# Attention, Fourier mixing and two MLPs on one core: some low-part subtractions change engine, and the first stage gets a new order

## The reference

```python
# 1. attention in chunks of 32 queries: 16 keys to the left, 32, 8 to the right, 8 memory keys; 8 heads of 64
scores = scale * np.matmul(q_c, k_full.transpose(0, 1, 3, 2))
scores = scores - np.max(scores, axis=-1, keepdims=True)
a = np.exp(scores)
a = a / (np.sum(a, axis=-1, keepdims=True) + 1e-09)
out[:, :, c_start:c_end] = np.matmul(a, v_full)
# 2. Fourier mixing and a channel MLP (d_model 512, hidden 2048)
mixed = np.real(fft(fft(x, axis=1), axis=2)).astype(np.float32)
u = x + mixed
un = (u - mu) / np.sqrt(var + 1e-06)
x = u + np.maximum(un @ w_ch1, 0.0) @ w_ch2
# 3. gated MLP with a convolution of 3 taps over the tokens (hidden 1024)
h = np.maximum(x @ w_in, 0.0)
return (h * sigmoid(conv3(h, conv_w))) @ w_out
```

## Time and profile before

| | |
|---|---|
| median of 3 runs | 959.13 us (956.21 to 959.7) |
| the profiled execution | 955.41 us, its span 953.6 us |
| PE busy | 923.5 us, 97% of the span |
| DVE, ACT, POOL busy | 679.6 us (71%), 419.3 us (44%), 178.3 us (19%) |
| chain that ended last | PE 86%, DVE 5%, DMA 3%, ScalarE 1%, GpSimd 1% |

### The profile page before, as it was taken

How to read it: one execution, slowest core, us unless ns; L and a number is a source line. 1 busy time by engine, 2 the same in 40 slices (tenths; PEclk the granted TensorE clock), 3 DMA queues, 4 the chain that set the end, 5 groups by cost and what they waited for, 6 DMA issues and landing times.

```text
span 953.6 us, 15306 instructions
## 1 busy us (share of the span) xinstructions
PE 923.5 (97%) x6072; PEld 828.7 (87%) x6072; DVE 679.6 (71%) x1205; ACT 419.3 (44%) x710; POOL 178.3 (19%) x233
## 2 busy tenths in 40 slices
PE   5899998989999999999999999999999999999998
PEld 4788888888988989989989899898898798998986
DVE  5758659796776755867737667276689699699693
ACT  3454557352343331452313523123366475575563
POOL 5985767213100010110100000100000000000000
PEclk9999999999999999999999999999999999999999
DMA  8967454487382853657555336665283272570301
GB/s 332 364 214 237 145 192 168 182 317 294 122 327 64 319 209 135 230 216 251 200 201 213 140 125 239 221 216 205 75 332 112 96 267 79 183 259 1 144 1 66
DMA packets 53782, 183.39 MB, mean 192 GB/s; under 512 B 8272, under 2 KB 14544, under 8 KB 46928
## 3 DMA queue, kind: packets, MB, share of 16 engines
q0 software_dynamic: 7776, 97.20, 27.4%
q1 hardware_dynamic: 45792, 85.16, 26.3%
q10 hardware_dynamic: 144, 0.07, 0.0%
HBM read 143.08 MB, written 39.32 MB: 191 GB/s over the span
## 4 chain that ended last, share of the span: by engine, by line
PE 86%; DVE 5%; DMA 3%; SPq 2%; ACT 1%; issue 1%; POOL 1%; DVEq 0%; POOLq 0%; ACTq 0%
PE ps L1049 35%; PE ps L1073 28%; PE ps L1463 12%; PE ps L545 5%; DMA k_win<-in_k 3%; PE ps L509 2%; PE ps L536 1%; PE ps L1328 1%; PE ps L1007 1%; SPq L259 1%; DVE conv_raw L1412 1%; PE ps L519 1%; PE ps L601 1%; DVE h_pad_raw L956 1%; SPq L249 1%
## 5 line engine op out<-in xcount | busy, mean ns | idle before, releaser
L1049 PE MATMUL ps<-x_hi,w 128*128 128x384 f32 x1344 | 344.6, 335 | 4.0 <-issue 2.2
L1073 PE MATMUL ps<-w,h 128*128 128x512 f32 x1152 | 268.1, 392 | 0.0
L1073 PEld LDWEIGHTS ps<-w,h 128*128 128x128 f32 x1152 | 215.3, 188 | 45.9
L1049 PEld LDWEIGHTS ps<-x_hi,w 128*128 128x128 f32 x1344 | 243.0, 188 | 5.4 <-issue 4.8
L1049 PE MATMUL ps<-x_lo,w 128*128 128x384 f32 x672 | 224.6, 334 | 0.0
L956 DVE TENSOR_TENSOR h_raw<-h_raw,ps 128x384 f32<-128x384 f32 x224 | 122.7, 553 | 60.4 <-PE ps L1049 50.4
L872 ACT ACTIVATE h<-h_raw 128x384 fp32r<-128x384 f32 x128 | 67.0, 526 | 155.7 <-DVE h_raw L956 153.7
L1049 PEld LDWEIGHTS ps<-x_lo,w 128*128 128x128 f32 x672 | 126.2, 188 | 0.5
L779 POOL DMA_DIRECT2D w<-w_scratch x40 | 21.2, 531 | 499.7 <-PE ps L1049 466.2
L1463 PE MATMUL ps<-w,h_pad 128*128 128x512 f32 x336 | 104.9, 393 | 0.0
L895 DVE TENSOR_TENSOR w<-w_raw,w 128x512 fp32r<-128x512 f32 x71 | 49.7, 710 | 44.3 <-ACT w L827 44.0
(11 more groups left out here) (114 smaller groups left out, 1199.9 us busy)
## 6 DMA issues: line engine op xcount, KB each, us to landing
w<-w_scratch POOLq DMA_DIRECT2D x40, 1792.0 KB, 7.9
w_raw<-in_moe_w SPq DMA_DIRECT2D x95, 256.0 KB, 2.9
w_scratch<-w POOLq DMA_DIRECT2D x12, 1792.0 KB, 7.1
v_win<-in_v SPq DMA_DIRECT2D x48, 260.0 KB, 4.4
k_win<-in_k SPq DMA_DIRECT2D x48, 256.0 KB, 4.6
q_sb<-in_q SPq DMA_DIRECT2D x24, 256.0 KB, 4.1
y_scratch<-u SPq DMA_DIRECT2D x8, 768.0 KB, 5.3
y_in<-y_scratch SPq DMA_DIRECT2D x4, 1536.0 KB, 7.9
```

Of the source, the lines that this page charges most:

```text
L1049: last = nc.tensor.matmul(result(n, i), a, b, start=(k == 0), stop=(k == 5))
L1073: last = nc.tensor.matmul(ps[:, t, :], h[:, m, part, cols], w2[j % R2][:, weight], start=(m == 0 and i == 0), stop=(m == GROUP - 1 and i = ...
```

## The change

1. In batch 0 the six subtractions `lower0.0` to `lower0.5` move from GpSimd's list to VectorE's. They get their own function, with the same wait on the high part. Those of batches 1 to 3 stay on GpSimd.
2. The low parts of the weights of the first three expansions (`blocks1(0..2)` and `sums1(0..2)`, six subtractions) move from VectorE's list to GpSimd's, as mlp6 to mlp11.
3. The four lists get a new order. TensorE starts `seq0.0` after `values0.4`, ahead of `scores1.1` and `values0.5`; the scores and values of batch 1 come later between the `seq` steps. ScalarE and VectorE follow. From `seq1.5` on, TensorE's list differs in one place only (`turn3.0` ahead of `scores3.2`). At the end of the stage ScalarE runs `split3.5` after mlp14 and `bh3.1`, mlp8 (`sums1(1)`) and `qs3.0` ahead of mlp6, and mlp9 (`sums1(2)`) ahead of `qs3.1`; VectorE runs `cm3.0` ahead of mlp10.

```diff
 "tensor"
-        "values0.2 turn0.3 scores0.5 values0.3 turn0.4 scores1.0 turn0.5 values0.4 scores1.1 turn1.0 "
-        "values0.5 seq0.0 scores1.2 values1.0 seq0.1 turn1.1 seq0.2 values1.1 seq0.3 scores1.3 seq0.4 turn1.2 "
-        "seq0.5 values1.2 scores1.4 dim0.0 turn1.3 seq0.6 values1.3 seq0.7 scores1.5 turn1.4 scores2.0 "
-        "values1.4 dim0.1 turn1.5 scores2.1 values1.5 mix0.0 turn2.0 mix0.1 scores2.2 mix0.2 turn2.1 mix0.3 "
+        "turn0.3 values0.2 scores0.5 values0.3 turn0.4 scores1.0 turn0.5 values0.4 seq0.0 scores1.1 seq0.1 "
+        "values0.5 seq0.2 turn1.0 seq0.3 scores1.2 turn1.1 scores1.3 values1.0 scores1.4 turn1.2 seq0.4 "
+        "values1.1 seq0.5 turn1.3 values1.2 scores1.5 dim0.0 turn1.4 seq0.6 turn1.5 seq0.7 values1.3 "
+        "scores2.0 scores2.1 values1.4 dim0.1 values1.5 turn2.0 scores2.2 mix0.0 turn2.1 mix0.1 values2.0 "
...
 "scalar"
-        "mirror2.0 bh2.6 bh2.7 keep3.5 qs2.1 split3.3 mirror2.1 split3.4 mlp1 mlp18 bh3.0 split3.5 mlp14 "
-        "bh3.1 mlp2 bh3.2 mlp3 bh3.3 mlp19 bh3.4 mlp7 bh3.5 mlp15 mlp5 mlp8 mlp4 mlp6 qs3.0 bh3.6 mirror3.0 "
-        "bh3.7 mlp16 mlp10 qs3.1 mlp9 mlp11 mirror3.1 mlp12 mlp13 "
+        "mirror2.0 bh2.6 bh2.7 keep3.5 qs2.1 split3.3 mirror2.1 split3.4 mlp1 mlp18 bh3.0 mlp14 bh3.1 "
+        "split3.5 mlp2 bh3.2 mlp3 bh3.3 mlp19 bh3.4 mlp7 bh3.5 mlp15 mlp5 mlp4 mlp8 qs3.0 mlp6 bh3.6 "
+        "mirror3.0 bh3.7 mlp16 mlp10 mlp9 qs3.1 mlp11 mirror3.1 mlp12 mlp13 "
 "vector"
-        "shift0.0 shift0.1 norm0.0 shift0.2 shift0.3 norm0.1 shift0.4 norm0.2 tablo0.0 shift0.5 norm0.3 "
-        "shift1.0 tablo0.1 norm0.4 shift1.1 norm0.5 tablo0.2 bl0.0 shift1.2 norm1.0 bl0.1 bl0.2 norm1.1 bl0.3 "
+        "shift0.0 shift0.1 norm0.0 shift0.2 shift0.3 norm0.1 lower0.0 shift0.4 norm0.2 tablo0.0 lower0.1 "
+        "shift0.5 norm0.3 lower0.2 tablo0.1 norm0.4 shift1.0 lower0.3 bl0.0 shift1.1 lower0.4 norm0.5 bl0.1 "
+        "tablo0.2 shift1.2 bl0.2 lower0.5 norm1.0 bl0.3 shift1.3 bl0.4 norm1.1 shift1.4 bl0.5 norm1.2 "
...
-        "norm3.4 mk2.0 mk2.1 norm3.5 mk2.2 mk2.3 mk2.4 mk2.5 mlp5 bl3.0 bl3.1 mlp7 bl3.2 mlp8 bl3.3 mlp20 "
-        "bl3.4 mlp13 bl3.5 mlp11 mlp21 mlp10 cm3.0 mlp12 bl3.6 mlp14 bl3.7 mlp16 cm3.1 mlp17 mk3.0 mlp22 "
-        "mk3.1 mlp15 mk3.2 mk3.3 mlp18 mk3.4 mlp19 mk3.5 "
+        "mk2.3 mk2.4 mk2.5 mlp5 bl3.0 bl3.1 mlp7 bl3.2 mlp8 bl3.3 bl3.4 bl3.5 mlp11 cm3.0 mlp10 mlp12 bl3.6 "
+        "bl3.7 mlp16 cm3.1 mlp17 mk3.0 mk3.1 mk3.2 mk3.3 mlp18 mk3.4 mlp19 mk3.5 "
 "gpsimd"
-        "table0.0 fold0.0 lower0.0 fold0.1 table0.1 fold0.2 lower0.1 fold0.3 lower0.2 fold0.4 lower0.3 "
+        "table0.0 fold0.0 fold0.1 table0.1 fold0.2 fold0.3 fold0.4 fold0.5 fold1.0 fold1.1 lower1.0 fold1.2 "
...
-        "lower3.3 fold3.4 fold3.5 lower3.4 lower3.5 mlp0 mlp1 mlp2 "
+        "lower3.0 lower3.1 fold3.2 lower3.2 fold3.3 lower3.3 fold3.4 fold3.5 lower3.4 lower3.5 mlp0 mlp6 mlp1 "
+        "mlp9 mlp7 mlp10 mlp2 mlp8 mlp11 "
 on VectorE, attention_and_fourier
+            def lower(b, j):
+                dve.wait_ge(z_hi_ready, b * TILES + j + 1)
+                nc.vector.tensor_tensor(of_unit(z_lo, j), of_unit(z_raw, j), of_unit(z_hi, j).bitcast(F32), ALU.subtract
+                                        ).then_inc(z_lo_ready, 1)
 on_gpsimd, channel_mlp
+        def lower1(n, part, ready):
+            rounded, plain = first_weights(n)
+            nc.gpsimd.tensor_tensor(rounded[:, part, 1], plain[:, part, 1], raw(rounded[:, part, 0]), ALU.subtract
+                                    ).then_inc(ready, 1)
+        def blocks1(n):
+            pool.wait_ge(a1_hi_ready, n + 1)
+            pool.wait_ge(s_ready, n + 1)
+            lower1(n, BLOCKS, a1_ready)
+        def sums1(n):
+            pool.wait_ge(s1_hi_ready, n + 1)
+            lower1(n, SUMS, s1_ready)
 first_gpsimd
         if k == 2:
             store_w1(pool, 0)
-        on_gpsimd(pool)(k)
+        if k < 3:
+            sums(k)
+        else:
+            (blocks1, sums1)[(k - 6) // 3](k % 3)
```

More of the change, by code:

```diff
@@ L482, in _ @@
                     lower_table(t)
+                elif step == "lower":
+                    lower(b, t)
                 elif step == "shift":
@@ L809, in sums @@
             nc.gpsimd.tensor_tensor(part(S4), part(A12), part(S2), ALU.subtract).then_inc(s_ready, 1)
-        return sums
+        def lower1(n, part, ready):
[9 more added lines that the diff above has]
+            lower1(n, SUMS, s1_ready)
+        return sums, blocks1, sums1
     def on_scalar(act):
@@ L1082, in first_gpsimd @@
     def first_gpsimd(pool, k):
+        sums, blocks1, sums1 = on_gpsimd(pool)
         if k == 2:
             store_w1(pool, 0)
-        on_gpsimd(pool)(k)
+        if k < 3:
+            sums(k)
+        else:
+            (blocks1, sums1)[(k - 6) // 3](k % 3)
     def first_scalar(act, k):
@@ L1163, in _ @@
         def _(pool):
-            sums = on_gpsimd(pool)
+            sums = on_gpsimd(pool)[0]
             for n in range(1, PAIRS):
```

## The result

The changed kernel takes 962.72 us (median of 6 runs, 960.65 to 964.93), the kernel before 958.20 in the same comparison. The ratio is 1.0053, with a 95% interval of 1.0033 to 1.0073, so +5.1 us (+3.2 to +7.0). It is inside the range of the prediction, and three times the +1.6 us of its sum. The profiled execution took 962.78 us against 955.41 before, so its span holds more of the loss than the medians do: 961.0 against 953.6, +7.4.

The account below looks back on a forecast made before the run. TensorE, busy 923.5 of 953.6 us, was taken to bound the kernel. The terms -0.74 + 0.15 + 0.4 + 2.2 - 0.4 sum to +1.6 us, giving 960 us, range 954 to 965.

Parts of the forecast that it names:

- The stake: TensorE's idle time in the stretches from 20 to 209.1 us: about 14.7 us, 1.5% of the time, is all to gain.
- The early order: `seq0.0` fills TensorE's gap before 37.70, -0.74 us; `turn0.5` comes late behind `lower0.1` and `split0.2`, +0.15 us (0 to +0.7).
- the first sign that was named for being right: TensorE's first `seq` starts at about 34.4, with no wait at `scores1.1`.
- part 2: VectorE and GpSimd operations with two SBUF inputs wait for each other and go in turns.
- The loads: Tile loads behind later value loads on SyncE: tiles 1.5 and 2.2 come 0.9 and 1.3 us late, +0.4 (0 to +2.2).
- The hold of VectorE: Near 167 us, GpSimd's long weight subtractions hold VectorE's mlp10 and mlp12 in turns; `expand(0)` then starts near 173, not 169.9.
- Rival A: GpSimd's long operations don't hold VectorE: `expand(0)` at 169.6, `mix3.0` at 179.5, total 956.4 us; chance 0.30.
- part 1: The prediction's step on the early order, with VectorE's six new subtractions of 128x512 at 710 ns, 4.3 us in all.
- the late term: End of the stage, from `dim3.0` to `mix3.0` as one chain: `mix3.0` later by +2.2 us (-1.35 to +3).
- The wait at 193.00: TensorE's wait of 1.87 us behind `mix3.0` shrinks because L960 is no longer held: -0.4 us (0 to -0.4).
- Rival C: Loads take over about 8 us, tiles 1.5 and 2.2 come 2.5 and 3 us late: +6.2, 964.6 us; chance 0.12.
- Rival B: Clearly faster: the early order fills most of the 5.5 us idle before 37.7; about 6 us less, 952.4; chance 0.12.

Follow-up runs that it names:

- The exchange on ScalarE: The changed lists up to batch 2, the kernel before's behind, with `exp0.5` ahead of `split0.2` on ScalarE: +1.8 us (+0.7 to +3.1) against the kernel before.
- early half: Everything up to `seq1.5`; run alone, the changed lists up to batch 2 with the kernel before's behind them: +3.4 us (+2.2 to +4.6) against the kernel before.
- experiment 3: The changed kernel with `values1.3` ahead of `seq0.6` on TensorE: +5.5 us (+3.9 to +7.0) against the kernel before.
- pieces: The late half alone with GpSimd's weight subtractions cut into instructions of 256 elements: -0.4 us (-1.1 to +0.5) against the kernel before.
- the late half alone: The kernel before's lists up to batch 2, the changed ones behind, weights' low parts on GpSimd: +3.7 us (+2.3 to +5.2) against the kernel before.
- three small moves at the end: The kernel before with `bl3.5` ahead of mlp13, mlp21 behind `bl3.6`, mlp11 ahead of mlp9, no engine changed: -1.6 us (-3.0 to -0.3), 954.66 us.

## Why the prediction was right, and where it was thin

**The stake** was read rightly: all of the difference arose between 20 and 200 us and nothing behind. Of the 14.7 us of idle in it neither half gained anything, and the versions that did gain took 1.3 to 1.6. The number was in part luck: 962.7 lies in a range of 11 us, but the sum was +1.6 and the interval of the measured +5.1 begins at +3.2. The direction and the main mechanism were right; three terms were too small.

**The early order, -0.74 + 0.15 us.** This term failed, and with it the first sign that was named for being right: `seq0.0` did not start at 34.4 but at 37.44. The term took `shift0.5` behind `lower0.1` and `exp0.5` behind `split0.2` for 0.15 us (0 to 0.7), and TensorE waited 2.89 us there. The walk took the fold of tile 0.2 to end where it had ended before, near 30.3. It ended at 33.3. `turn0.3` ahead of `values0.2`, which the walk had no term for, is 1.1 of the 2.5 us by which the fold started late; the rest were keys that came 0.7 us later and a low clock in this execution. On top, VectorE's new subtraction held GpSimd's second addition (0.4 us), a hold that part 2 had described and the walk then left out. The exchange on ScalarE took back half of the early half's loss.

**The loads, +0.4 (0 to +2.2).** The mechanism was named and the place was right (tile 2.2), the size not: 2.84 us. Of these 1.3 stand in the prediction's own working, for a landing of 6.4 us. The load was issued 3.6 us later than said (69.68, not 66.1) and wanted 2.5 later (73.70, not 71.2), which makes 1.1, and it landed in 6.9 us, which makes 0.5. Most of the early term's delay thus cancels. For tile 1.5 the sum has a slip: 48.5 and 6.4 give 54.9 and not 55.6, so 0.2 us late; it came in time. What was missed is that mending this load gains nothing measurable (experiment 3).

**The hold of VectorE.** Right in mechanism, turns and place. In before's clock (less 4.46) `expand(0)` began at 172.5 where 173 was said, `dim3.0` at 161.0 where 161.5, `mix3.0` at 184.2 where 183.1. L949, now L970, took 6.09 us for its pair. What the Trainium skill says in "SBUF — State Buffer", section "Terms" (the shared port pair is held for the full instruction, and the loser is blocked), is borne out for GpSimd instructions of 1.8 to 2.4 us too: long instructions gave 6.09, pieces 3.10, none 2.35. Rival A, no hold at all, is refuted. GpSimd's price was estimated at 1.93 and 2.52 us; the 768 took 1.83, the mean over both shapes, holds included, is 2.28. (The 710 ns of part 1 for a subtraction of 128x512 on VectorE is 699 in the earlier trace rows; nothing turns on it.)

**What the late term lacked** is the clock: 1.7 us of the 3.4 are matmuls at a granted clock of 0.57 after a wait of 4.16. The prediction had the wait right (173 less the end of `seq3.7` near 169, so 4) and counted it as the whole cost: it has `mix3.0` 10.1 us behind the start of `expand(0)`, and it came 11.68 behind.

**The wait at 193.00, -0.4,** came as said (1.87 to 1.45). **Rival C** was right about the direction of the loads and wrong about the cause: the keys of tile 2.2 took 6.9 us and not 8, the issue was late. Its sign, a wait for keys over 1 us between 50 and 75 us, was met: the wait of 2.84 us began at 73.70. **Rival B** had no support anywhere.

The bound that the prediction sets between "same" and "slower", 0.5%, is 4.8 us; the measured +5.1 (+3.2 to +7.0) can't be put on either side of it. The chance of 0.12 for the slower side was too low for a sum whose early part rested on a long walk through the lists.

## What to carry to other kernels

Before you move a two-input subtraction to GpSimd because it is idle, look for what VectorE must do with two SBUF inputs at the same time, and who waits for that: each of these can wait for a whole GpSimd instruction. If the work must go there, cut it into short instructions; here that turned +3.7 us into -0.4. In a list that is written by hand, an engine's step that waits for a slow producer should not stand ahead of one on the path of the busiest engine; the exchange of two such steps took the early half from +3.4 to +1.8, though the intervals overlap. And the three small moves at the end, with no engine changed, gained 1.6 us where the whole redistribution lost 5.1.

## What the runs showed of the hardware

Where VectorE and GpSimd both had operations with two SBUF inputs queued, they took turns, one instruction each, also when GpSimd's took 1.8 to 2.4 us: two of VectorE's 1.22 us took 6.09, and 3.10 beside GpSimd's pieces of 0.7. The stall shows as duration and not as idle time on either engine. After a wait of TensorE of 4.16 us the granted clock was 0.57 over the next 4 us (a mean of the levels of 1.2 and 2.4 GHz); 30 matmuls took 7.04 us in the changed kernel and 7.65 in the late half alone, instead of 5.37. After a wait of 1.16 us they took 5.48.
